# Two expert layers behind a short convolution: where the routing steps of the next pass stand in a tile, what computes their reciprocals, and when the second half's tap exponentials run

## The reference

```python
# 1. a causal convolution of 7 taps; the taps are a softmax per token and head (8 heads of 24 values)
w = exp(weight_gen - max(weight_gen, -1)); w = w / (sum(w, -1) + 1e-9)
tok = einsum('bshk,bskhg->bshg', w, x_unf)          # x_unf: each token and the six before it

# 2. eight experts, two for each token, picked by noisy scores
noisy = tok @ w_gate + log1p(exp(tok @ w_noise)) * noise
top2 = the two largest of noisy;  share = softmax over the two
y = sum over the two of share * (max(tok @ w1[e], 0) @ w2[e])      # w1: 192x1024, w2: 1024x192

# 3. eight experts, one for each token
e = argmax(y @ w_gate2);  out = softmax(y @ w_gate2)[e] * (max(y @ w1_2[e], 0) @ w2_2[e])
```

## Time and profile before

| | us |
|---|---|
| median of 3 runs | 1223.77 (1223.09 to 1226.0) |
| the profiled execution | 1223.26 |
| its span, first to last instruction | 1221.5 |

### The profile page before, as it was taken

How to read it: one execution, slowest core, us unless ns; L and a number is a source line. 1 busy time by engine, 2 the same in 40 slices (tenths; PEclk the granted TensorE clock), 3 DMA queues, 4 the chain that set the end, 5 groups by cost and what they waited for, 6 DMA issues and landing times.

```text
span 1221.5 us, 28357 instructions
## 1 busy us (share of the span) xinstructions
PE 1097.5 (90%) x8218; PEld 1059.8 (87%) x8219; DVE 789.2 (65%) x1350; ACT 532.6 (44%) x1037; POOL 527.7 (43%) x621
## 2 busy tenths in 40 slices
PE   3962899999899999999989999998999888999996
PEld 1641789999899999999988999998999888999995
DVE  9998689996686544555576545546655864655642
ACT  2240334554442444467344434445753433454432
POOL 1000465665343554444445545544453433555542
PEclk9985899999999999999999999999998989999998
DMA  7142132234522334622226333356432473443510
GB/s 244 52 162 64 52 84 70 83 82 144 145 73 81 94 106 138 220 69 84 82 68 205 93 101 83 106 169 201 128 101 64 132 216 99 114 147 106 138 45 22
DMA packets 97780, 136.47 MB, mean 112 GB/s; under 512 B 25994, under 2 KB 75981, under 8 KB 97484
## 3 DMA queue, kind: packets, MB, share of 16 engines
q1 hardware_dynamic: 78284, 92.96, 25.9%
q0 software_dynamic: 19456, 43.04, 12.0%
HBM read 104.74 MB, written 34.54 MB: 114 GB/s over the span
## 4 chain that ended last, share of the span: by engine, by line
PE 59%; DVE 18%; issue 9%; DMA 7%; ACT 2%; DVEq 2%; POOL 1%; ACTq 0%; POOLq 0%; SPq 0%; PEldq 0%
PE ps_y L1467 16%; PE ps_y L1468 7%; DMA row<-x_rows,read_now 6%; PE ps_h L1437 6%; PE ps_h L1441 6%; PE ps_h L1447 6%; PE ps_h L1444 6%; PE ps_h L1438 5%; DVE prod L590 3%; DVE h_lo L905 2%; PE ps_x L1423 2%; DVE prod L602 1%; PE ps_x L1424 1%; PE ps_route L1371 1%; DVE prod L791 1%
## 5 line engine op out<-in xcount | busy, mean ns | idle before, releaser
L1467 PE MATMUL ps_y<-w_hl,h_hi 128*128 128x384 f32 x1480 | 450.6, 368 | 12.8 <-DVE h_lo L905 11.7
L905 DVE SCALAR_TENSOR_TENSOR h_lo<-ps_h,h_hi 128x512 fp32r<-128x512 f32 x404 | 258.9, 685 | 254.8 <-ACT h_hi L1214 213.2
L1468 PE MATMUL ps_y<-w_hl,h_lo 128*128 128x192 f32 x1480 | 373.4, 252 | 0.0
L1214 ACT ACTIVATE h_hi<-ps_h 128x512 fp32r<-128x512 f32 x404 | 219.5, 595 | 307.0 <-PE ps_h L1447 295.1
L1467 PEld LDWEIGHTS ps_y<-w_hl,h_hi 128*128 128x128 f32 x1480 | 281.8, 190 | 17.8 <-DVE h_lo L905 16.5
L1468 PEld LDWEIGHTS ps_y<-w_hl,h_lo 128*128 128x128 f32 x1480 | 286.3, 193 | 0.0
L486 POOL DMA_INDIRECT row<-x_rows,read_now x202 | 229.7, 1137 | 119.6 <-POOL read_now L482 81.0
L1437 PE MATMUL ps_h<-xa_hi,w1a_hi 128*128 128x256 f32 (+1 forms) x808 | 236.1, 292 | 10.0 <-issue 5.1
L1441 PE MATMUL ps_h<-xa_lo,w1a_hi 128*128 128x256 f32 (+1 forms) x808 | 232.0, 287 | 11.5 <-DVE xa_lo L894 11.5
L1447 PE MATMUL ps_h<-xb_lo,w1b_hl 128*128 128x256 f32 (+1 forms) x808 | 231.9, 287 | 0.0
L1444 PE MATMUL ps_h<-xb_hh,w1b_hl 128*128 128x256 f32 (+1 forms) x808 | 230.4, 285 | 0.0
(11 more groups left out here) (183 smaller groups left out, 1266.9 us busy)
## 6 DMA issues: line engine op xcount, KB each, us to landing
w_raw<-in_moe_w_dram SPq DMA_DIRECT2D x32, 768.0 KB
w1a_raw<-in_moe_w_dram SPq DMA_DIRECT2D x32, 512.0 KB
w1b_raw<-in_moe_w_dram SPq DMA_DIRECT2D x64, 256.0 KB
x_pad<-in_x_dram SPq DMA_DIRECT2D x2, 2688.0 KB, 10.6
x_pad<-y_rows SPq DMA_DIRECT2D x14, 384.0 KB
prod<-y_rows SPq DMA_DIRECT2D x14, 384.0 KB
x_rows<-tok SPq DMA_DIRECT2D x4, 1344.0 KB
row<-x_rows,read_now POOLq DMA_INDIRECT x202
```

The costliest lines, as they stand in the source:

```text
L905: nc.vector.scalar_tensor_tensor(out=h_lo[:, i * GF:(i + 1) * GF, :], in0=ps_h[:, i, :].rearrange("p (f t) -> p f t", f=GF), scalar=0.0, i ...
L1214: act.activation(h_hi[:, i * GF:(i + 1) * GF, :], ps_h[:, i, :].rearrange("p (f t) -> p f t", f=GF), ACT.Relu).then_inc(h_hi_ready, 1)
L1467: nc.tensor.matmul(ps_y[:, u, 0:2 * D], h_hi[:, i, cols], w2_hl[b][:, f, :], start=(i == 0), stop=False)
L1468: last = nc.tensor.matmul(ps_y[:, u, 0:D], h_lo[:, i, cols], w2_hl[b][:, f, 0:D], start=False, stop=(i == FC - 1))
```

## The change

- In the convolution the plain product is made first in each block, and its operand goes first on TensorE: order 3, 0, 1, 2.
- `soft(1)` on ScalarE moves from the last block to behind `logarithm(0)`. `softmax_divide(1)` on VectorE moves from behind `softmax_shift(1)` to behind `list_rows(0)`, in front of the first tile's `split_rows`.
- `logarithm` ends with the logarithm. VectorE makes the reciprocal from `d_lane` (`invert_exps`): at once in the front, and for pass 1 in tile 16 ahead of its `split_rows`.
- The two choices are cut into two parts each. In pass 0 `noisy_values`, `choose_first`, `rank_tokens`, `place` 0 and 2, the second half of `mark_some` and `list_rows` now stand in `before_results`, behind `split_rows`; `choose_first` moves to tile 17, `choose_second` and `rank_tokens` to tile 18, and all from `COUNT` on by one tile (`COUNT[0]` is 19, so that `LIST[0]` is 23).
- In passes 1 and 2, `choose_first` is one part ahead of `split_rows` and one behind; `place` 0 and 2, the second half of `mark_some` and `list_rows` move behind it; `shares` moves from behind it in the tile after the count to ahead of it in the tile of the count, and the first part of `scale_tokens` goes from before the `h_lo` of one tile to behind those of the tile before.

```diff
+    CONV_ORDER = (*range(PAIRS, OPERANDS), *range(PAIRS))
...
-        COUNT = (SCORE[0] + 3, SCORE[1] + 1, SCORE[2] + 1)
+        COUNT = (SCORE[0] + 4, SCORE[1] + 1, SCORE[2] + 1)
...
                 for g in blocks:
+                    for slot in range(PAIRS, OPERANDS):
+                        slot_free(g, slot)
+                        product(g, slot + PAIRS, slot).then_inc(conv_ready, 1)
                     for slot in range(PAIRS):
...
                     add_pair(g, PAIRS - 1)
-                    for slot in range(PAIRS, OPERANDS):
-                        slot_free(g, slot)
-                        product(g, slot + PAIRS, slot).then_inc(conv_ready, 1)
...
+            def invert_exps(p):
+
+                dve.wait_ge(scored[p], 4)
+                nc.vector.reciprocal(both[:, :, :], d_lane[:, :, :]).then_inc(inverted, 1)
 
             def noisy_values(p):
...
-                dve.wait_ge(scored[p], 6)
+                dve.wait_ge(scored[p], 5)
...
+                dve.wait_ge(inverted, p + 1)
...
             def before_splits(p, j):
...
-                if p == 0 and j == SCORE[p] + 2:
-                    choose_second(q)
+                if p == 0 and j == SCORE[p] + 3:
+                    choose_second(q, 0)
                 if j == COUNT[p] + 1:
                     place(q, 1)
                 if p > 0 and j == COUNT[p] + 2:
-                    scale_tokens(q, 0)
                     scale_tokens(q, 1)
...
             def after_splits(p, j):
+
+                q = p + 1
+                if p == 0 and j == SCORE[p] + 1:
+                    invert_exps(q)
+                if p == 0 and j == SCORE[p] + 3:
+                    choose_second(q, 1)
+                if p > 0 and j == SCORE[p]:
+                    choose_first(q, 0)
+                if p > 0 and j == COUNT[p]:
+                    shares(q)
+                if p > 0 and j == COUNT[p] + 1:
+                    scale_tokens(q, 0)
+                if p > 0 and j == COUNT[p] + 2:
+                    scale_tokens(q, 2)
+
+            def before_results(p, j):
 
                 q = p + 1
                 if p == 0 and j == SCORE[p] + 1:
                     noisy_values(q)
                 if p == 0 and j == SCORE[p] + 2:
+                    choose_first(q, 0)
+                    choose_first(q, 1)
+                if p == 0 and j == SCORE[p] + 3:
                     rank_tokens(q)
                 if p > 0 and j == SCORE[p]:
-                    choose_first(q)
+                    choose_first(q, 1)
+                    rank_tokens(q)
                 if j == COUNT[p]:
                     place(q, 0)
                 if j == COUNT[p] + 1:
                     place(q, 2)
                 if p > 0 and j == COUNT[p] + 2:
-                    scale_tokens(q, 2)
+                    scale_tokens(q, 3)
                 if MARK[p] <= j < LIST[p]:
                     mark_some(p, j, 1)
                 if j == LIST[p]:
                     list_rows(q)
-
-            def before_results(p, j):
...
             softmax_shift(1)
-            softmax_divide(1)
             split_w1a(0, 0)
...
+            invert_exps(0)
             noisy_values(0)
...
             list_rows(0)
+            softmax_divide(1)
             split_rows(0)
...
-                    if (c, g) == (0, NB - 1):
-                        soft(1)
                     evacuate(c, g)
...
-                act.wait_ge(scored[p], 5)
-                act.activation(both[:, :, :], value[:, :, :], ACT.Exp, scale=-1.0).then_inc(scored[p], 1)
...
             logarithm(0)
+            soft(1)
             read_counts(0)
...
-                for i in range(OPERANDS):
+                for i, slot in enumerate(CONV_ORDER):
```

More of the change, by code:

```diff
@@ L204, in build @@
         turns_read = [sem(f"turns{q}_read") for q in range(PASSES)]
+        inverted = sem("inverted")
         scored_cols = [sem(f"scored_cols{q}") for q in range(PASSES)]
@@ L597, in slot_free @@
                     if c * NB + g > 0:
-                        dve.wait_ge(conv_used, (c * NB + g - 1) * OPERANDS + slot + 1)
+                        dve.wait_ge(conv_used, (c * NB + g - 1) * OPERANDS + CONV_ORDER.index(slot) + 1)
                 def add_pair(g, slot):
@@ L645, in noisy_values, with choose_first, choose_second @@
                 step(nc.vector.tensor_tensor(value[:, :, :], value[:, :, :], logit[:, :, 0:E], ALU.add))
-            def choose_first(p):
-                step = stepper(dve, f"first_step{p}")
-                if p >= C:
-                    dve.wait_ge(scored[p], 1)
-                    step(nc.vector.tensor_copy(value[:, :, :], logit[:, :, 0:E]))
-                first_of_max(step, best1, hot1)
-            def choose_second(p):
-                step = stepper(dve, f"second_step{p}")
-                step(nc.vector.scalar_tensor_tensor(out=value[:, :, :], in0=hot1[:, :, :], scalar=-BIG, in1=value[:, :, :],
-                                                    op0=ALU.mult, op1=ALU.add))
-                first_of_max(step, best2, hot2)
-                step(nc.vector.tensor_tensor(both[:, :, :], hot1[:, :, :], hot2[:, :, :], ALU.add))
+            def choose_first(p, part):
+                step = stepper(dve, f"first_step{p}_{part}")
+                if part == 0:
+                    if p >= C:
+                        dve.wait_ge(scored[p], 1)
+                        step(nc.vector.tensor_copy(value[:, :, :], logit[:, :, 0:E]))
+                    mark_below(step, best1, hot1)
+                else:
+                    mark_first(step, hot1)
+            def choose_second(p, part):
+                step = stepper(dve, f"second_step{p}_{part}")
+                if part == 0:
+                    step(nc.vector.scalar_tensor_tensor(out=value[:, :, :], in0=hot1[:, :, :], scalar=-BIG, in1=value[:, :, :],
+                                                        op0=ALU.mult, op1=ALU.add))
+                    mark_below(step, best2, hot2)
+                else:
+                    mark_first(step, hot2)
+                    step(nc.vector.tensor_tensor(both[:, :, :], hot1[:, :, :], hot2[:, :, :], ALU.add))
             def rank_tokens(p):
@@ L954, in after_splits @@
                     list_rows(q)
-            def before_results(p, j):
-                q = p + 1
-                if p == 0 and j == SCORE[p] + 1:
-                    choose_first(q)
-                if p > 0 and j == SCORE[p]:
-                    rank_tokens(q)
-                if p > 0 and j == COUNT[p] + 1:
-                    shares(q)
-                if p > 0 and j == COUNT[p] + 2:
-                    scale_tokens(q, 3)
                 if p == 0 and j == LIST[p]:
@@ L1026, in _ @@
             dve.reg_mov(buffer_ahead, 0)
+            invert_exps(0)
             noisy_values(0)
-            choose_first(0)
-            choose_second(0)
+            for part in range(2):
+                choose_first(0, part)
+            for part in range(2):
+                choose_second(0, part)
             rank_tokens(0)
@@ L1313, in convolve @@
                         last = nc.tensor.matmul(ps_h[:, 2 * (g % 2) + half, 0:BLOCK // 2], ident[:, :],
-                                                prods[:, i, half * (BLOCK // 2):(half + 1) * (BLOCK // 2)],
+                                                prods[:, slot, half * (BLOCK // 2):(half + 1) * (BLOCK // 2)],
                                                 start=(i == 0), stop=(i == OPERANDS - 1))
```

9 lines of the change are left out of this document (5 added, 4 removed).

## The result

| | before | after |
|---|---|---|
| median of 6 runs, us | 1224.88 (1219.58 to 1228.12) | 1207.32 (1204.35 to 1210.09) |
| the profiled execution | 1223.26 | 1204.87 |
| its span | 1221.5 | 1203.1 |

After by before is 0.9859 [0.9827, 0.989]: 17.6 us faster by the medians and 18.4 by the two profiled executions, where 19.2 were forecast. The time forecast was 1204.1. The six runs of after fall into three near 1204.5 and three near 1210, and those of before lie 8.5 us apart, so a single run of either kernel says little under 6 us.

What follows compares the result with a forecast made beforehand. TensorE's matmuls were taken to bound from 128 us, VectorE only where late; before that, one chain. Gains of 4.3 + 6.4 + 3.7 + 5.3 less 0.5 make 19.2, from 1223.3 to 1204.1 us, range 1198 to 1211.5.

Steps and rivals of the forecast that it cites:

- Front: Before the first tile: block order, exponentials and reciprocal bring the first routing step 4.6 us earlier; 4.3 after GpSimd's price.
- GpSimd beside the divide: Front: the moved divide may slow GpSimd's list copy and gather issue, between 0 and 1.1 us, taken as 0.3.
- Pass 0: Routing tiles of pass 0: waits of 5.7 us and a clock loss of 1.7 go, 1.0 stays: 6.4 us.
- the term of 1.7 for the clock: Pass 0, tiles with waits: the fall to 1.2 GHz behind them goes, gaining 1.7 us.
- Pass 1: Routing tiles of pass 1: of 6.7 us of waits 3.0 stay, so 3.7 us gained.
- no `xa_lo` wait over 0.7: All passes, a sign of success: no TensorE wait for `xa_lo` longer than 0.7 us.
- Pass 2: Routing tiles of pass 2: waits only move, 10.6 against 10.0 us; the clock's recovery gives 5.3 us.
- the 4.2 of the clock: Pass 2, behind the first choice's wait: 10.3 us at 1.2 GHz go, worth 4.2 us.
- New cost: Count tile's `share_exps`: its exponential may need a table load in each pass; 0.5 us together for passes 1 and 2.
- slower: the table: Rival: up to three table loads in each pass 0 tile cost 26 us, giving 1230 us; chance 0.03.
- VectorE is the bound: Rival, routing tiles: steps moved off `xa_lo` delay `y` and the next `h_lo` equally; 1209.6 us, chance 0.18.
- New waits throw the clock: Rival: uncovered clock falls behind new 3 us waits, or late gathers, give back 4 to 7 us; 1209 to 1211, chance 0.10.

Runs made afterwards that it cites:

- `after_third`: After's code unchanged, run again on another chip: median 1203.48 us, 0.9858 of before.
- `front_only`: After with the routing steps of all passes and the later reciprocal as in before, so only the front changed: median 1215.5 us, 0.9961 of before.
- `exp_on_scalar`: After with pass 1's reciprocal made on ScalarE again as exp(-ln): median 1203.51 us, 0.9879 of before.
- `best`: After with steps of passes 0 and 1 spread over more tiles and pass 1's reciprocal on ScalarE again: 1196.0 us, 0.9787 of before.
- `best_pass2_old`: `best` with the steps that stand in pass 2 placed as in before: 1201.85 us, 0.9829 of before.

## Why the prediction was right, and where not

The forecast of 1204.1 held (1207.3 by the median, 1204.87 in the profiled execution), and so did its picture, that the waits for `xa_lo` go and part of them comes back as waits for `h_lo`. By its own steps:

- **Front, 4.3 forecast, 5.4 to the first `xa_lo` in after.** The transposes came 2.4 us earlier where 2.2 were forecast, and the order's own part, 1.3, measured 1.2 to 1.5; the second table load and its exponential went as said, with a reciprocal of 1.55 (I took 1.5). Two terms were off. The last scores escaped 1.2 GHz fully in after (0.7 counted, 1.3 got) and not at all in `after_third`. Over the twelve traces with the moved exponentials seven escaped fully, four in part and one not, so that half was somewhat too little even as a mean. The ten traces with the whole of the new front gain 4.2 to 5.7 to the first tile. And GpSimd beside the divide, at 0.3, was nothing: its copy took 0.18 us beside the reduction, as with VectorE idle in before (0.19).

```profile
115.51 0.18 POOL L484 COPY read_now<-read_from 128x2 int32<-128x2 int32 x1 [110.65 <-DVE write_to L796]
116.58 1.04 POOL L488 DMA_INDIRECT row<-x_rows,read_now  x1 [0.88 <-POOL read_now L484]
```

  The Trainium skill ("VectorE: DVE Perf Modes", "Two Vector instructions with no wait between them") ties the sharing to operations with two SBUF inputs. The trace agrees: the copy ran beside reductions, the multiplications came at 118.89, after the issue.
- **Pass 0, 6.4 forecast, 7.2 to 8.4 measured in the twelve traces with the new places.** The waits left are 1.4 (forecast 1.0), so the extra gain isn't there. And the term of 1.7 for the clock was no gain of its own. `front_only` has the old places and is at 2.4 GHz all through tiles 15 to 31, and it takes as long for them as before (+0.1), and for the tile of the fall, number 17, 14.3 us in both. Where before has its 3.4 us at 1.2 GHz, TensorE waits for `h_lo` instead:

```profile
322.22 0.45 PE L1492 MATMUL ps_y<-w_hl,h_hi 128*128 128x384 f32 x1 [2.11 <-DVE h_lo L924]
```

  VectorE's steps bounded that tile at either clock, and moving them is what gave the time: the waits for `h_lo` and `xa_lo` in tiles 15 to 31 are 8.1 us in `front_only` and 1.4 in after. What the sum has as waits and clock, 7.4, was 8.1 of waiting for VectorE, partly covered by the slower matmuls. TensorE's busy time over these tiles is 158.9 in `front_only` and 157.7 in after; that 1.2 I can't place. The remainder of 0.2 in tile 16 was not there at all, and by `exp_on_scalar` the reciprocal decides only a few tenths.
- **Pass 1, 3.7 forecast, 3.3 to 4.5 measured in tiles 41 to 63.** The new wait at `place` 1 is 1.50 against 1.4. The first choice kept 1.12 and not 0.5: "three steps and a copy stay ahead" was the step mis-sized, and "no `xa_lo` wait over 0.7" fell with it. That holds for four of the eight traces with after's steps there; in the other four 0.3 or nothing is left, and they are all at 1.2 GHz for 3.4 to 6.8 us at or just ahead of that tile.
- **Pass 2, 5.3 forecast, 2.0 in the profiled execution, 1.2 and 6.7 in two more of the same code.** The waits are mostly as walked: 0.65, 3.0, 2.4, 2.4, 1.5 forecast, 0.73, 3.40, 1.52, 2.39, 1.29 measured, and the 0.7 for `w1b_hl` between them not there; together 9.3 where 10.6 were forecast and before had 10.0. The failed term is the 4.2 of the clock (with the 1.7 of one more fall). I took it that the fall goes with the shorter wait. It came in 4 of 10 traces behind the same wait, and in after all of tiles 63 to 80 is at 1.2 GHz for as long as before, 23.9 us, so that the term gave nothing. It should have stood as two outcomes; the gains of 0.8 to 2.2 with a fall and 3.6 to 6.7 without are wide enough to make most of the spread between the runs of after. That its mean was not far off, the ten traces with the new places show (3.6 gained on average, and the three with the old ones lose 1.1) and `best` against `best_pass2_old`, 5.9 us.
- **New cost, 0.5.** The wrong step. "Five table loads or a few more" was one load per pass by my sum, and it became 48, the mechanism of the rival "slower: the table", which had a chance of 0.03. Its trigger happened: the loads stand in front of a Relu, in the tiles of pass 0 that run before the logarithm as well as behind it. Its price did not: one load a tile, not three, and in pass 0 ScalarE hides it. In pass 1 it costs about 2.4 us, 3 with the falls of the clock, and not 0.5. The argument against it, that the trace of before has no such load, held only for a kernel in which each logarithm is followed by an exponential.
- Of the rivals, *VectorE is the bound* would have given pass 0 4.6 and pass 1 1.3: out in every trace with the new places. In pass 2 its picture held, as in the prediction's own walk: the waits moved and hardly shrank. *New waits throw the clock* is half true: one fall of 3.4 us came behind the wait at 939.33, and in seven of the nine traces in which this wait is 3.2 to 3.4 us long the clock fell at its end or within 1.6 us behind it, for 3.4 to 6.8 us.

In the profiled execution the parts are 5.7 to the first `y_lo`, 7.7 in pass 0, -1.8 at the start of pass 1, 3.3 in the rest of it, 2.0 in pass 2 and 1.5 in pass 3: 18.4. Forecast were 4.3, 6.4, -0.5, 3.7, 5.3 and nothing: 19.2. Too little in the front and pass 0 made up for too much in pass 2; the total was closer than its terms. That is luck in part: nothing was changed in pass 3, and its 1.5 are the clock's, which fell for 3.4 us there in before and not at all in this execution of after.

## What to carry to other kernels

When steps move behind the operands that TensorE waits for next, walk the queue of the engine on to the next thing that it owes: the waits that came back were where the walk put them (3.40 for 3.0, 1.50 for 1.4), and spreading the steps over more tiles removed them (5 to 6 us more, in three traces). An activation function that ends a rarely taken branch can put a table load in front of all that may run behind it, as it did in all five kernels here that end so; if its table isn't the usual one, put the usual one back there with an exponential of one column, and count the table loads in the trace. Where a wait and a fall of the clock stand in one tile, the fall may be hiding a longer wait, so that taking it away gives nothing (2.11 us of wait came in its place in `front_only`). A term that hangs on whether the clock falls is two outcomes, and belongs in the range, not in the sum.

## What the runs showed of the hardware

- **Table loads.** 1283 ns each. A logarithm and an exponential behind it still load twice (83.69 and 85.39). The Trainium skill ("ScalarE: Activation LUTs", "Table sets: the hidden batching unit") says that one set holds both and that cheap functions such as Relu are in every set. Which functions a set holds no trace shows; as far as loads go the trace disagrees with both: there is one in front of each of the two, and 48 stand in front of a Relu. They appear in all seven traces of kernels whose later logarithm is the last function of its branch, and in none of the six (nor in before) where an exponential follows it.
- That the placement is made ahead of the run, for a stretch of code which may be reached with either table, is argued from this and not shown. The Trainium skill ("ScalarE activation tables: per-element evaluation and per-set limits", "Table sets in the compiler and the runtime") says that the loads are placed per block; no run here looked at it.
- **The clock.** It fell behind a wait of 0.73 us in four traces and not in six others, and behind after's wait of 3.40 us at 939.33 for 3.4 us only. It is at 1.2 or 2.4 GHz, and rows of one execution can't tell which it will be in the next.
- **Reciprocals on VectorE** grow in full with the columns: 0.33 us for 28, 0.82 for 112, 1.55 for 224.
